# Splitting one accumulation of a fused attention and MoE kernel into two halves of its columns

## The reference

```python
logits = x @ phi                       # [3072, 32]
d = exp(logits - logits.max(0)); d /= d.sum(0)
slot_input = d.T @ x                   # the dispatch: [32, 512]
slot_out[e] = relu(slot_input[e] @ w1[e]) @ w2[e]
out = softmax(logits, axis=1) @ slot_out
```

## Time and profile before

| what | us |
|---|---|
| median of 3 runs | 465.17 |
| lowest, highest | 465.12, 467.6 |
| the profiled execution's own time | 469.86 |
| its span, first to last instruction | 467.9 |

### The profile page before, as it was taken

One profiled execution on the slowest core, in us unless ns is written; L12 is line 12 of the kernel. 1 busy time (PEld: TensorE's weight loads), 2 busy tenths in 40 slices (PEclk: granted clock), 3 DMA queues, 4 the chain that ended last, 5 costly groups with the idle time before them and its releaser, 6 DMA issues.

```text
span 467.9 us, 12260 instructions
## 1 busy us (share of the span) xinstructions
PE 448.6 (96%) x5438; PEld 332.6 (71%) x5438; DVE 276.7 (59%) x540; ACT 138.9 (30%) x257; POOL 47.4 (10%) x44
## 2 busy tenths in 40 slices
PE   6799999999999999999999999999999999999990
PEld 5699777777876787767777777787677878543560
DVE  4567558765596566766665785568644557541142
ACT  2475233232331322332332323323222222210031
POOL 2576000000000000000000000000000000010000
PEclk9899999999999999999999999999999999999997
DMA  8996232321142143303321132130160479999997
GB/s 293 411 415 276 101 117 88 104 91 54 59 193 72 37 188 102 103 2 102 104 97 49 59 102 61 46 133 1 30 242 0 182 284 424 395 420 422 420 399 295
DMA packets 14820, 81.59 MB, mean 174 GB/s; under 512 B 1584, under 2 KB 1712, under 8 KB 8880
## 3 DMA queue, kind: packets, MB, share of 16 engines
q1 hardware_dynamic: 14768, 80.81, 45.0%
HBM read 74.51 MB, written 6.29 MB: 173 GB/s over the span
## 4 chain that ended last, share of the span: by engine, by line
PE 92%; DMA 3%; DVE 2%; issue 1%; ACT 0%; DVEq 0%
PE h_ps L310 57%; PE o_ps L294 5%; PE lpu_ps L327 5%; PE sx_ps L269 4%; PE lpu_ps L360 4%; DMA qk_sb<-qk 3%; PE sx_ps L360 2%; PE pt_ps L280 2%; PE sx_ps L699 2%; PE h_ps L1013 2%; PE lpu_ps L699 2%; PE h_ps L734 1%; PE h_ps L951 1%; PE o_ps L993 1%; PE lpu_ps L370 1%; PE pt_ps L1013 1%
## 5 line engine op out<-in xcount | busy, mean ns | idle before, releaser
L310 PE MATMUL h_ps<-x_odd,w_pair 128*128 128x512 f32 x576 | 138.3, 394 | 0.0
L310 PEld LDWEIGHTS h_ps<-x_odd,w_pair 128*128 128x128 f32 x576 | 106.3, 188 | 27.8 <-issue 4.6
L545 DVE SCALAR_TENSOR_TENSOR gT<-gT,h_ps 128x512 f32<-128x512 f32 (+1 forms) x108 | 66.1, 612 | 93.1 <-ACT gT L427 93.0
L427 ACT ACTIVATE gT<-h_ps 128x512 f32<-128x512 f32 (+1 forms) x108 | 58.4, 541 | 178.1 <-PE h_ps L310 177.4
L310 PE MATMUL h_ps<-x_even,w_pair 128*128 128x512 f32 x384 | 92.5, 395 | 0.0
L310 PEld LDWEIGHTS h_ps<-x_even,w_pair 128*128 128x128 f32 x384 | 70.9, 188 | 16.8 <-issue 1.7
L555 DVE STREAM_TRANSPOSE gB<-gT 128x512 f32<-128x512 f32 x80 | 56.7, 709 | 1.8
L310 PE MATMUL h_ps<-x_short,w_pair 128*128 128x256 f32 x384 | 51.6, 288 | 1.0 <-DVE gT L545 0.5
L310 PEld LDWEIGHTS h_ps<-x_short,w_pair 128*128 128x128 f32 x384 | 47.7, 192 | 6.0 <-issue 3.6
L529 POOL TENSOR_TENSOR sc<-sc,row_stats 128x512 f32<-128x512 f32 x23 | 24.0, 1044 | 275.0 <-DVE row_stats L523 275.0
L447 ACT ACTIVATE sc<-sc 128x512 f32<-128x512 f32 x23 | 14.6, 633 | 53.2 <-DVE sc L512 49.1
(11 more groups left out here) (193 smaller groups left out, 383.6 us busy)
## 6 DMA issues: line engine op xcount, KB each, us to landing
unit<-w SPq DMA_DIRECT2D x31, 1024.0 KB, 9.6
qk_sb<-qk SPq DMA_DIRECT2D x24, 640.0 KB, 5.4
v_sb<-v SPq DMA_DIRECT2D x24, 512.0 KB, 3.6
out<-unit SPq DMA_DIRECT2D x6, 1024.0 KB, 7.2
w_stage<-w_in SPq DMA_DIRECT2D x4, 1024.0 KB, 12.0
wot<-w_outT SPq DMA_DIRECT2D x4, 1024.0 KB, 12.7
unit<-w_out SPq DMA_DIRECT2D x4, 1024.0 KB, 5.3
unit_acc<-w SPq DMA_DIRECT2D x1, 1024.0 KB, 8.7
```

The costliest lines, as they stand in the source:

```text
L310: last = nc.tensor.matmul(h_ps[k % 2][:, 0:TOKS[b]], w_pair[:, k // 2, w, kc, k % 2 * 128:k % 2 * 128 + 128], x[:, lo, kc, 0:TOKS[b]], sta ...
L427: nc.scalar.activation(gt_of(b, k), h_ps[k % 2][:, 0:TOKS[b]], ACT.Tanh, scale=0.5).then_inc(tanh_done, 1)
L545: nc.vector.scalar_tensor_tensor(out=gt_of(b, k), in0=gt_of(b, k), scalar=1.0, in1=h_ps[k % 2][:, 0:TOKS[b]], op0=ALU.add, op1=ALU.mult).t ...
```

## The change

The dispatch of block 5 is made in two halves. The first sums quarters 1 and 2 of the columns (places 9 and 10) over all four rounds and raises a new semaphore `u_half`; the second sums quarters 0 and 3 (places 8 and 11) and raises `u_mm`. Each half has 64 matmuls of 256 columns instead of 64 of 512 for the whole. The loads into places 9 and 10 wait for `u_half` instead of `u_mm`; their order in the queue is the same.

```diff
+            if b == LAST - 1:
+                for half, quarters in enumerate((slice(1, 3), slice(0, 4, 3))):
+                    for r in range(rounds):
+                        for c in range(4):
+                            for i in range(4):
+                                j, rows = 4 * r + c, slice(32 * i, 32 * i + 32)
+                                slots = gB[rows, 4:20, 32 * j:32 * j + 32].rearrange("p (a s) t -> p a s t", a=4)
+                                sums = u_ps[i][32 * c:32 * c + 32, :].rearrange("p (a f) -> p a f", a=4)
+                                last = nc.tensor.matmul(sums[:, quarters, :], eB[rows, 32 * j:32 * j + 32],
+                                                        slots[:, quarters, :, :], start=(r == 0), stop=(r == rounds - 1))
+                    last.then_inc(u_mm if half else u_half, 1)
+                return
...
-                places += [(i, u_mm, NB - 1) for i in (9, 10, 11)]
+                places += [(9, u_half, 1), (10, u_half, 1), (11, u_mm, NB - 1)]
```

More of the change, by code:

```diff
@@ L216, in moe_program @@
         total_done, et_done, raw_kept, u_mm, acc_done = sem("total_done"), sem("et_done"), sem("raw_kept"), sem("u_mm"), sem("acc_done")
+        u_half = sem("u_half")
         tail_dve, stored = sem("tail_dve"), sem("stored")
```

## The result

The changed kernel took 468.67 us (median of 17 runs, 466.94 to 469.93), the kernel before 465.81 us (17 runs, 464.32 to 467.74). The ratio is 1.0058, interval 1.0045 to 1.0071: 0.58% slower, 2.7 us. The forecast was 466.0 us, a range of 464.5 to 467.5, and "no change".

What follows compares the result with a forecast made beforehand. The prediction took PE's chain through block 5's dispatch as the bound, with a nearly full DMA queue. It added +0.8 us for the dispatch and 0 for the loads to 465.17 us: 466.0 us, range 464.5 to 467.5.

Steps and rivals of the forecast that it cites:

- what bounds the kernel: Block 5's dispatch on PE: chunk 5 and DVE's additions wait behind it, so its +0.8 us lies on the path whole.
- the streaming: Time the dispatch's columns take through the PE tiles: 3.44 us, unchanged by twice the records of half the columns.
- the joins: Pauses between rounds of the dispatch, about 0.20 us each; 7 instead of 3, so +0.8 us, dispatch 5.2 us.
- the once-paid part: In the dispatch, the spread of a burst and the way out of the array: 0.36 us, paid once.
- Rival B: Pauses between the dispatch's rounds halve with the records' columns: +0.1 us, down to -0.6; 464.6 to 465.3 us; chance 0.17.
- where the lead goes: DMA queue: places 9 and 10 issued 1.8 us earlier, all of it lost at 407 us before places 7 and 8.
- Rival C: The earlier loads' 1.8 us reaches the last store: 464.2 us, at best 462.4; chance 0.08.
- can the instructions themselves become the bound?: Dispatch's 256 records at the scores' 13.4 ns each need 3.4 us, no more than streaming; count not taken as bound.
- the 6.7 that the forecast named as its sign of being wrong: Length of block 5's dispatch: the prediction is wrong if it takes 6.7 us or more.
- The upper bound of 8.8 us: Longest dispatch allowed: 256 records at 34 ns each, +4.4 us.
- an even price: Every dispatch record costs the same whatever its columns: up to +4.4 us, taken as 466.7 to 469.6 us; chance 0.13.
- The rule of about 25 ns: Skill's minimum spacing of matmul starts: dispatch some 6.8 us, +2.4, kernel 467.6 us; set aside for the trace's rows.

Runs made afterwards that it cites:

- the two halves apart: Against the changed kernel, chunk 5 of block 6 was put between the two halves of the dispatch; measured 1.0044 (1.0019 to 1.0069) of the kernel before.
- quiet queue: Against the changed kernel, places 14 and 15 were loaded behind 9, 10 and 11, so no load was under way at the dispatch's start; 469.4 us, one run.
- the run with quarters: Against the changed kernel, block 5's dispatch was made in four quarters of 128 columns, 512 records, 1024 PE instructions; one run of 478.5 us.

## Why the prediction was wrong, by its own steps

**Right: what bounds the kernel.** PE's chain runs through the dispatch, and every microsecond of it comes out at the end: +2.60 in the dispatch, +2.53 at the last copy, about +2.7 measured.

**Right: the streaming and, nearly, the joins.** A round of halved records is 0.65 us, 0.43 and 0.22. With joins of 0.22 instead of 0.20 us the same sum gives 5.3 us for a row without a pause, not 5.2: this term is about +0.9 instead of +0.8. (The 5.51 us of the two halves apart pay the once-paid part twice.) What a tile waits for at a join wasn't tested. Rival B is out.

**Right in the outcome, not in the place: where the lead goes.** It was real (the slices of 0 are gone), it never reached the end, and taking it away changed nothing measurable. But the queue was not full up to 406.8 us, and of 0.66 MB only 0.07 were left after 20 us, not all of it up to 407 us. Rival C is out.

**Wrong: "can the instructions themselves become the bound?"** This is the step that failed. I took the scores' 64 records in 0.86 us as the price at which records can be issued, and multiplied by 256. But 64 records are 128 instructions. They say how fast PE goes through code that is at hand, not how fast more code comes. In a row of 512 dense instructions, a border comes at which PE has used up its code, and it stood still for 1.2 us by the timeline, 1.7 us by the difference of 7.00 and the estimated 5.3. So the sum lacked a term: +0.8 was forecast, +2.60 measured, and the pause is nearly all of what lies between. The dispatch's 7.00 us is also past the 6.7 that the forecast named as its sign of being wrong. The upper bound of 8.8 us held the 7.00, but I gave it 0.13 and named another mechanism, an even price. With +2.6 instead of +0.8 the forecast would have been 467.8 us by the same sum. Of the rest of the distance to 468.67 us, 0.64 is the starting point: the sum began at 465.17 us, three runs of the kernel before, and its 17 runs beside the changed one gave 465.81.

The Trainium skill has the border. "Runtime: NRT & Kernel Launch", section "Instruction fetch mechanics", says that code comes in blocks of 256 instructions over a DMA queue of its own. The runs agree: the pause moves back to its record with 256 instructions more, and comes every 128 records when supply is the bound. The same section of the Trainium skill says that crossing a border is mostly hidden. The trace agrees outside the dense row: from 20 us on PE has no other wait for "issue" of over 0.2 us. In a row of 512 a border cost 1.7 us. That section of the Trainium skill also says that PE holds 2048 instructions. The runs don't bear that out: PE stopped 362 instructions into the row and went on some 2.4 us after a packet of code had started. The rule of about 25 ns that I weighed (the Trainium skill's "TensorE: Matmul & The Clock Gate", section "Wait — 56ns, not 53.3ns?") gave about the right time, 467.6 us, for a reason that the trace doesn't show: in the bursts two records start every 0.03 us (374.36, 374.39), and then comes one long gap.

**Shown, and not.** Shown: the pause belongs to the code's borders (moved by 128 and 256 instructions), it is gone with a slow chunk inside the row, there are more pauses with more instructions (quarters), and in one run with a quiet queue it was 0.16 us. Only argued: that the code packet waits on the same DMA engines as the loads. I have its start times, the empty queue and the two packets of the run with quarters, not its way through the engines. Open: why it takes some 2.4 us from the packet's start until PE goes on, and when the packet is asked for.

## What to carry to other kernels

Before splitting small matmuls, count the instructions in a row, not only their columns: here a row of 256 PE instructions that took 4.4 us was free, and rows of 512 and 1024 ran dry, the more so while large loads filled the queue; so did 256 tiny ones behind other dense code. A wait whose releaser is "issue", in the middle of a row of matmuls, is the sign; moving the code by a few dozen tiny instructions shows whether a border is the cause. And before releasing a transfer earlier, look at what releases the ones behind it: here PE did, no earlier than before, and the lead was gone within 20 us.

## What the runs showed of the hardware that was not expected

- PE stood still for 1.20 us in a row of 512 instructions, and for 2.76, 1.22 and 3.39 us in a row of 1024, which came in parts of 128 records.
- A row of 256 instructions, the whole dispatch of 4.40 us, showed no pause in any profile; the 256 instructions of tiny matmuls, with one column each, showed one of 1.42 us.
- A packet of code started 1.7 us into the dispatch with an empty queue, and 2.8 to 3.0 us into it with loads of 1 MB under way; the first record behind the pause followed some 2.4 us later each time (2.3 to 2.6 us in the row of 1024).
- After PE's pause of 2.76 us the granted clock was 0.63 of full speed over the next stretch and 0.50 in the two behind it.
